# A float32 attention and two-MLP kernel: weight sums and splits moved from GpSimd to VectorE and ScalarE, y loads moved ahead of weight loads

## Chip, core and metric

One core of a Trainium2 chip. The metric is device time in microseconds, the median of several executions of one program. All values are float32; every product is made from split operands.

## What is computed

```python
# x: (8, 8, 512, 64), state: (8, 8, 32, 64)   (batch, head, token, width)
xread = softmax(x @ state.T / 8) @ state          # 8 batches x 512 tokens
sread = softmax(state @ x.T / 8) @ x              # 8 batches x 32 state tokens
x = concat([xread, sread], axis=2)                # as rows: 4608 tokens x 512
x = relu(x @ w_in) ** 2 @ w_out                   # 512 -> 2048 -> 512
out = ((x @ w1) * (x @ w2)) @ w3 @ w_out2         # 512 -> 1024 -> 1024 -> 512
```

## The kernel before

A float32 operand is split into two parts that TensorE takes at full rate: `hi`, a copy rounded to float32r (made by ScalarE), and `lo`, the whole minus `hi` (made by VectorE). A product is three matmuls, hi x hi, hi x lo, lo x hi.

The work has three stages.

Start: `w3 @ w_out2` is folded into one matrix W', and state and `w_in` into a table G, both written to DRAM.

First block, once for each batch tile t = 0 to 7 of 512 tokens (GpSimd's stores of y mark the ends of the tiles), and once more, as tile `SR` with 256 columns, for all the state tokens. A tile has 16 chunks f of the hidden width. For each chunk TensorE makes `h(f)` in a PSUM bank, ScalarE takes the relu (L1050), VectorE squares it (`h_chunk`, L1315 to L1320), ScalarE rounds the square to `v_hi`, VectorE subtracts to get `v_lo` (`minus`), and TensorE adds `y(f)` into four PSUM banks. TensorE runs `h` two chunks ahead of `y`: its order is h(f+2), a piece of the next batch's attention in some chunks, y(f). Beside each chunk, in a slot written out by hand (`in_slot`, `attention_slot`, `tile_slots`), ScalarE and VectorE carry on the softmax of the next batch and split the next pieces of x and G, which SP loads into a ring of 8 buffers `raw`; SP issues a load when the piece that held the buffer 8 pieces earlier is split. A batch tile splits 16 such pieces. Chunk and tile counts gate everything through semaphores.

Second block: `(x @ w1) * (x @ w2) @ W'` with a Strassen-like scheme of 7 products on 2 x 2 blocks. Its weights are sums of blocks of `w1` and `w2`; each of the sums is split too, and stands in `s_dram` (`s_scratch`), 8 kinds for each of 4 groups. In the kernel before GpSimd makes all of these: `S_weights(g)` (L609 to L645) loads four blocks of 128 x 512 into `top_f`, and for each kind copies with rounding into `top[:, 5]` (L627), subtracts into `top[:, 6]` (L620), and stores both as one DMA of 512 KB (L631), waiting for the last store before it overwrites the pair; 4 more operations are sums. `S_weights(0)` to `(3)` stand behind the stores of y of tiles 1 to 4, so they run beside tiles 2 to 5.

Between the blocks, in tile `SR`, SP loads the second block's weights (`load_S`) as the buffers they go to come free, then y of tile 0 into `raw` (`load_y`, L521), then the first four rows of W' (`load_wp`, L524). VectorE makes the column sums of y (`T_sums`, in slot 9), and 7 sets of y columns are rounded and split in slots 10 to 13 (`set_slots`), the 8 rows of W' in slots 14 and 15 (`wp_slots`). W' rows 4 to 7 are loaded into the ring buffers of rows 0 to 3. The second block's first chunk needs all sets, the weights of groups 0 and 1, the relu of the last chunk of `SR`, and, from its fifth product on, ScalarE's copy `P1`, which stands behind the rounding of W' rows 4 to 7 in ScalarE's program.

Of the kernel before, what the change touches and what calls it, by code (L numbers as in the profile page):

```python
# [34 lines left out]
def build_program(nc, x_tok, x_T, state_T, moe_w_in, moe_w_out, moe2_w1, moe2_w2, w3_T, moe2_w_out, out):  # L35
# [21 lines left out]
    RAW_AT = 4736  # L57
    TOP_AT = 214144
# [8 lines left out]
    SHIFT = 80  # L67
# [15 lines left out]
    with ctx:  # L83
# [49 lines left out]
        top_f = nc.alloc_sbuf_tensor_at("top_f", [P, N_SETS, C], F32, offset=TOP_AT)  # L133
# [19 lines left out]
        def sr(a):  # L153
# [10 lines left out]
                      .rearrange("p (j k n) -> p j k n", j=N_SETS, k=2)[:, :, :, 0:HT] for t in (X_hi, X_lo))  # L164
# [14 lines left out]
        def rest_bank(m):  # L179
# [11 lines left out]
                v_rows + [raw_r[:, k] for k in range(3)]]  # L191

        def A_block(g, row, col):

            half, kk = g // 2, g % 2
            c = 2 * col + kk
            return (moe2_w1, moe2_w2)[row][c * P:(c + 1) * P, half * C:(half + 1) * C]
# [53 lines left out]
        S_step = sem("S_step")  # L251
        S_stored = sem("S_stored")
# [113 lines left out]
        set_slots = {10: [0], 11: [1, 2], 12: [3, 4], 13: [5, 6]}  # L366
# [104 lines left out]
        def _(sp):  # L471
# [10 lines left out]
            def tile(b, slot_lists, r0, i=0):  # L482
# [26 lines left out]
            with sp.Fori(0, (NB - 2) // 2) as i:  # L509
                tile(2 * i + 1, tile_slots, R_1, i)  # L510
                tile(2 * i + 2, tile_slots, R_1 + PT, i)
# [21 lines left out]
            sp.wait_ge(S_stored, 16 * 4 * KINDS)  # L533
# [46 lines left out]
        def _(pool):  # L580
# [6 lines left out]
            last.then_inc(bd_zero, 1)  # L587
            nc.gpsimd.memset(ident[:], 1.0).then_inc(ones_ready, 1)
# [20 lines left out]
            def S_weights(g):  # L609
                A11, A12, A21, A22, S3 = (top_f[:, k] for k in range(5))  # L610
                n = g * (4 + 2 * KINDS)
                stores = g * KINDS
                for dst, row, col in ((A11, 0, 0), (A12, 0, 1), (A21, 1, 0), (A22, 1, 1)):
                    pool.dma_start(dst, A_block(g, row, col)).then_inc(A_loaded, 16)
                pool.wait_ge(A_loaded, 16 * 4 * (g + 1))

                def total(dst, a, b, op):
                    nonlocal n
                    wait_for(pool, S_step, n)
                    nc.gpsimd.tensor_tensor(dst, a, b, op).then_inc(S_step, 1)  # L620
                    n += 1

                def split(src, j):
                    nonlocal n, stores
                    wait_for(pool, S_stored, 16 * stores)
                    wait_for(pool, S_step, n)
                    nc.gpsimd.tensor_copy(top[:, 5], src).then_inc(S_step, 1)  # L627
                    n += 1
                    total(top[:, 6], src, top[:, 5].bitcast(F32), ALU.subtract)
                    pool.wait_ge(S_step, n)  # L630
                    pool.dma_start(s_dram[g, j].rearrange("k p n -> p k n"), top[:, 5:7].bitcast(F32)).then_inc(S_stored, 16)  # L631
                    stores += 1

                split(A11, 0)
                split(A21, 7)
                total(S3, A11, A21, ALU.subtract)
                split(S3, 2)
                total(A21, A21, A22, ALU.add)
                split(A21, 3)
                split(A22, 5)  # L640
                total(A11, A21, A11, ALU.subtract)
                split(A11, 1)
                split(A12, 4)
                total(A12, A12, A11, ALU.subtract)
                split(A12, 6)  # L645

            store_y(0, S)
            for g in range(4):
                store_y(g + 1, S)
                S_weights(g)  # L650
            for t in range(5, NB):
                store_y(t, S)
# [306 lines left out]
        def _(act):  # L959
# [87 lines left out]
            def h_chunk(t, n, f):  # L1047
                act.wait_ge(h_full, KF * t + f + 1)
                wait_for(act, sq_done, KF * t + f - 1)
                nc.scalar.activation(t1[:, f % 2, 0:n], ps_h[:, f % 2, 0:n], ACT.Relu).then_inc(relu_done, 1)  # L1050
                wait_for(act, y_full, KF * t + f - 3)
# [3 lines left out]
            def first_block(t, n, in_slot, next_chunk, next_slot):  # L1055

                for f in range(2, KF):
                    h_chunk(t, n, f)
# [116 lines left out]
            with act.Fori(0, (NB - 4) // 2) as i:  # L1175
                b = 2 * i + 1
                slot_b1 = batch_slot(b + 1, 0, tile_slots, R_1 + PT, i)
                first_block(b, S, batch_slot(b, 1, tile_slots, R_1, i), h_of(b + 1, S), slot_b1)
                first_block(b + 1, S, slot_b1, h_of(b + 2, S),
                            batch_slot(b + 2, 1, tile_slots, R_1 + 2 * PT, i))  # L1180
# [16 lines left out]
        def _(dve):  # L1197
# [117 lines left out]
            def h_chunk(t, n, f):  # L1315
                dve.wait_ge(relu_done, KF * t + f + 1)
                relu = t1[:, f % 2, 0:n]
                tt(t2[:, f % 2, 0:n], relu, relu, ALU.mult).then_inc(sq_done, 1)
# [194 lines left out]
```

## Time and profile before

| | us |
|---|---|
| median of 3 runs | 1301.54 (1298.03 to 1304.68) |
| the profiled execution | 1298.76 |
| its span in the profile | 1297.2 |

```profile
span 1297.2 us, 19431 instructions
## 1 busy us (share of the span) xinstructions
PE 1248.2 (96%) x7177; PEld 1083.0 (83%) x7177; DVE 835.7 (64%) x1397; ACT 476.6 (37%) x904; POOL 147.3 (11%) x164
## 2 busy tenths in 40 slices
PE   8979999999999989899999989999999999999998
PEld 6657888877877768778888989999999999999998
DVE  6666877678686786876554465666566665757541
ACT  6565554534445344454444231212122121212111
POOL 1000000044262442610000000000000000000000
PEclk9988999999999999999999999999999999999999
```

Each digit is a slice of 32 us. PE is TensorE, DVE VectorE, ACT ScalarE, POOL GpSimd. GpSimd has work in slices 9 to 18. The second block fills slices 24 to 40.

### The profile page before, as it was taken

Reading aid. Unit: us, or ns where it says so; the run is one execution under the profiler, and the core shown is the slowest. Engines: PE = TensorE matmul, PEld = TensorE weight load, DVE = VectorE, ACT = ScalarE, POOL = GpSimd, SP = SyncE. Lnnn points to the kernel's source line nnn. Section 1 sums busy time; section 2 is a strip of 40 time slices with the busy share of each in tenths; the row PEclk is TensorE's granted clock in tenths of the full one; section 3 lists DMA queues with packets and bytes.
Section 4 is the critical chain, followed back from the end, with each engine's and each line's share of the span. In section 5 each row is a group of like instructions: output and inputs, shape, how many; then the busy total and the mean of one; then the engine's idle time right before and its main releaser. Section 6 shows DMA issues by size and latency. Waiting matters only on the chain.

```text
span 1297.2 us, 19431 instructions
## 1 busy us (share of the span) xinstructions
PE 1248.2 (96%) x7177; PEld 1083.0 (83%) x7177; DVE 835.7 (64%) x1397; ACT 476.6 (37%) x904; POOL 147.3 (11%) x164
## 2 busy tenths in 40 slices
PE   8979999999999989899999989999999999999998
PEld 6657888877877768778888989999999999999998
DVE  6666877678686786876554465666566665757541
ACT  6565554534445344454444231212122121212111
POOL 1000000044262442610000000000000000000000
PEclk9988999999999999999999999999999999999999
DMA  8986431143433434331123770101010101010210
GB/s 297 363 295 210 137 129 55 64 155 135 141 129 122 145 120 130 130 126 59 42 98 122 252 266 11 66 1 65 0 65 0 65 0 65 3 61 0 82 50 33
DMA packets 63092, 139.10 MB, mean 107 GB/s; under 512 B 5184, under 2 KB 6208, under 8 KB 63040
## 3 DMA queue, kind: packets, MB, share of 16 engines
q1 hardware_dynamic: 51680, 96.49, 22.2%
q0 software_dynamic: 11360, 41.95, 9.2%
q8 instruction: 29, 0.48, 0.1%
q14 instruction: 23, 0.19, 0.0%
HBM read 84.93 MB, written 53.48 MB: 107 GB/s over the span
## 4 chain that ended last, share of the span: by engine, by line
PE 80%; DVE 11%; DMA 3%; ACT 3%; issue 2%; SPq 0%; DVEq 0%; ACTq 0%; POOL 0%; POOLq 0%
PE ps_y L674 39%; PE ps_h L674 21%; PE ps_t L674 18%; DVE t L1201 3%; ACT v_hi L964 2%; DVE GA L1201 1%; DVE s L1201 1%; DVE v_lo L1201 1%; DVE aT_lo L1201 1%; DMA g_scratch<-g_extra 1%; DMA wp_scratch<-stage 1%; DVE x_lo L1201 1%; DMA raw<-y_scratch 1%; DMA g_scratch<-stage 1%; PE ps_h L733 1%
## 5 line engine op out<-in xcount | busy, mean ns | idle before, releaser
L964 ACT CAST v_hi<-t 128x512 fp32r<-128x512 f32 (+1 forms) x216 | 128.9, 597 | 538.4 <-DVE t L1201 533.8
L674 PE MATMUL ps_y<-v_hi,X_hi 128*128 128x512 f32 (+1 forms) x576 | 223.3, 388 | 25.4 <-DVE v_lo L1201 23.1
L1201 DVE TENSOR_TENSOR v_lo<-t,v_hi 128x512 fp32r<-128x512 f32 (+1 forms) x216 | 150.3, 696 | 147.9 <-ACT v_hi L964 147.9
L674 PE MATMUL ps_y<-v_lo,X_hi 128*128 128x512 f32 (+1 forms) x576 | 219.9, 382 | 0.0
L674 PE MATMUL ps_y<-v_hi,X_lo 128*128 128x512 f32 (+1 forms) x576 | 219.2, 381 | 0.0
L1201 DVE TENSOR_TENSOR t<-t 128x256 f32<-128x256 f32 (+1 forms) x272 | 160.9, 611 | 83.9 <-ACT t L1050 81.5
L674 PEld LDWEIGHTS ps_y<-v_hi,X_hi 128*128 128x128 f32 x576 | 109.7, 190 | 52.9 <-DVE v_lo L1201 31.1
L674 PEld LDWEIGHTS ps_y<-v_hi,X_lo 128*128 128x128 f32 x576 | 109.9, 191 | 21.0
L1050 ACT ACTIVATE t<-ps_h 128x512 f32<-128x512 f32 (+1 forms) x144 | 82.3, 572 | 119.9 <-PE ps_h L674 119.4
L674 PEld LDWEIGHTS ps_y<-v_lo,X_hi 128*128 128x128 f32 x576 | 109.9, 191 | 19.1
L1201 DVE TENSOR_TENSOR t<-t,ps_t 128x256 f32<-128x256 f32 (+1 forms) x132 | 72.6, 550 | 48.1 <-PE ps_t L674 34.3
L674 PE MATMUL ps_h<-aT_hi,GA 128*128 128x512 f32 (+1 forms) x288 | 95.7, 378 | 0.5 <-ACT g_extra L964 0.5
L674 PE MATMUL ps_h<-aT_hi,GB 128*128 128x512 f32 (+1 forms) x288 | 95.6, 377 | 0.0
L674 PE MATMUL ps_y<-v_hi,GB 128*128 128x512 f32 (+1 forms) x288 | 91.6, 382 | 0.4 <-DVE v_lo L1201 0.4
L674 PE MATMUL ps_y<-v_hi,GA 128*128 128x512 f32 (+1 forms) x288 | 91.5, 381 | 0.0
L1201 DVE TENSOR_TENSOR t<-t,ps_h 128x256 f32<-128x256 f32 x132 | 55.0, 417 | 56.2 <-PE ps_h L674 44.2
L1201 DVE TENSOR_TENSOR t<-ps_t,t 128x512 f32<-128x512 f32 x64 | 44.2, 691 | 44.5 <-PE ps_t L674 43.7
L964 ACT COPY t<-ps_h 128x256 f32<-128x256 f32 (+1 forms) x74 | 31.5, 426 | 85.7 <-PE ps_h L674 81.9
L674 PEld LDWEIGHTS ps_h<-aT_hi,GA 128*128 128x128 f32 x288 | 53.3, 188 | 11.2 <-ACT g_extra L964 0.9
L674 PEld LDWEIGHTS ps_h<-aT_hi,GB 128*128 128x128 f32 x288 | 53.5, 189 | 10.1
L674 PEld LDWEIGHTS ps_y<-v_hi,GB 128*128 128x128 f32 x288 | 53.3, 188 | 10.3 <-DVE v_lo L1201 0.6
L1201 DVE TENSOR_TENSOR X_lo<-raw,X_hi 128x512 fp32r<-128x512 f32 x66 | 45.3, 687 | 25.0 <-ACT X_hi L964 24.9
(232 smaller groups left out, 2885.2 us busy)
## 6 DMA issues: line engine op xcount, KB each, us to landing
raw<-g_scratch SPq DMA_DIRECT2D x64, 256.0 KB
s_scratch<-top POOLq DMA_DIRECT2D x32, 512.0 KB, 3.8
raw<-in_moe_w_in SPq DMA_DIRECT2D x32, 256.0 KB
raw<-in_x_T SPq DMA_DIRECT2D x32, 256.0 KB
raw<-in_x_tok SPq DMA_DIRECT2D x32, 256.0 KB
y_scratch<-stage POOLq DMA_DIRECT2D x8, 1024.0 KB, 5.5
raw<-y_scratch SPq DMA_DIRECT2D x8, 1024.0 KB, 5.3
out<-stage POOLq DMA_DIRECT2D x8, 1024.0 KB, 4.6
```

The lines of the kernel that those rows point to most:

```text
L674: mm = nc.tensor.matmul(dst, w, m, start=first and n == 0, stop=last and n == 2)
L733: last = nc.tensor.matmul(pair_banks(p)[:, par, :], w[half, 0, par, rows], m[half], start=n == 0, stop=n == 2)
L964: return nc.scalar.copy(dst, src)
L1050: nc.scalar.activation(t1[:, f % 2, 0:n], ps_h[:, f % 2, 0:n], ACT.Relu).then_inc(relu_done, 1)
L1201: return nc.vector.tensor_tensor(dst, a, b, op)
```

## The change

1. GpSimd's `S_weights` goes. In `h_chunk` of tiles 1 to 4 a call `S_part(f, i, kk)` stands between the square and the low part on VectorE, and between the relu and the rounding of the square on ScalarE. In chunks 2, 3, 5, 7, 8, 10, 11 and 13 ScalarE rounds one kind and VectorE subtracts; in chunks 4, 6, 9 and 12 VectorE makes one sum. Each group takes one tile.
2. Two pairs of buffers are used in turn (`parts`: `top[:, 5:7]` and two rows of `E_lo`). GpSimd stores each part on its own, so 64 DMAs of 256 KB in place of 32 of 512 KB, and ScalarE waits for the stores two kinds back before it overwrites, and for all of them in chunk 15.
3. The loads of the blocks of `w1` and `w2` go from GpSimd's queue to SP's, behind the fourth piece of a tile, and behind a wait for the last split of the group before.
4. In SP's program the load of y tile 0 and of W' rows 0 to 3 goes ahead of the wait for the stored weights and of all `load_S`. `T_sums` goes from slot 9 to slot 8 of tile `SR`, set 0 to slot 9, and set 3 to slot 11.

```diff
+        parts = [(top[:, 5], top[:, 6]), (E_lo[:, 6], E_lo[:, 7])]
+        A11, A12, A21, A22, S3 = (top_f[:, k] for k in range(5))
+        work = {2: (A11, 0), 3: (A21, 7), 5: (S3, 2), 7: (A21, 3), 8: (A22, 5), 10: (A11, 1), 11: (A12, 4),
+                13: (A12, 6)}
+        total = {4: (S3, A11, A21, ALU.subtract), 6: (A21, A21, A22, ALU.add), 9: (A11, A21, A11, ALU.subtract),
+                 12: (A12, A12, A11, ALU.subtract)}
...
-        set_slots = {10: [0], 11: [1, 2], 12: [3, 4], 13: [5, 6]}
+        set_slots = {9: [0], 10: [1], 11: [2, 3], 12: [4], 13: [5, 6]}
...
+                    if kk is not None and n == 3:
+                        sp.wait_ge(S_split, i * 2 * KINDS + kk * KINDS + 1)
+                        for dst, row, col in ((A11, 0, 0), (A12, 0, 1), (A21, 1, 0), (A22, 1, 1)):
+                            sp.dma_start(dst, A_block(i, kk, row, col)).then_inc(A_loaded, 16)
...
-            sp.wait_ge(S_stored, 16 * 4 * KINDS)
+            sp.wait_ge(piece_split, N_RING)
+            sp.wait_ge(y_stored, 16)
+            load_y(y_main[0])
+            sp.wait_ge(wp_stored, 16 * 2)
+            for k in range(4):
+                load_wp(k)
+            for stored_part in S_stored:
+                sp.wait_ge(stored_part, 16 * 4 * KINDS)
             load_S(0, 1, range(N_SETS))
...
-            sp.wait_ge(piece_split, N_RING)
-            sp.wait_ge(y_stored, 16)
-            load_y(y_main[0])
-            sp.wait_ge(wp_stored, 16 * 2)
-            for k in range(4):
-                load_wp(k)
...
+            def store_S(i, kk):
+                for n, j in enumerate(order_S):
+                    pool.wait_ge(S_split, i * 2 * KINDS + kk * KINDS + n + 2)
+                    dst = s_dram.rearrange("(h k) j s p n -> h k j s p n", k=2)[i][kk, j]
+                    for part in range(2):
+                        pool.dma_start(dst[part], parts[n % 2][part].bitcast(F32)).then_inc(S_stored[n % 2], 16)
...
+            def S_part(f, i, kk):
+                if f in work:
+                    n = order_S.index(work[f][1])
+                    if n == 0:
+                        act.wait_ge(A_loaded, i * 2 * 64 + (kk + 1) * 64)
+                    if n > 1:
+                        act.wait_ge(S_stored[n % 2], i * 32 * KINDS + (kk * KINDS // 2 + n // 2) * 32)
+                    if f > 4:
+                        act.wait_ge(S_total, i * 8 + kk * 4 + (f > 4) + (f > 6) + (f > 9) + (f > 12))
+                    copy(parts[n % 2][0], work[f][0]).then_inc(S_rounded, 1)
+                if f == 15:
+                    for stored_part in S_stored:
+                        act.wait_ge(stored_part, i * 32 * KINDS + (kk + 1) * 16 * KINDS)
...
+            def S_part(f, i, kk):
+                if f == 2:
+                    dve.wait_ge(A_loaded, i * 2 * 64 + (kk + 1) * 64)
+                if f in work:
+                    n = order_S.index(work[f][1])
+                    dve.wait_ge(S_rounded, i * 2 * KINDS + kk * KINDS + n + 1)
+                    tt(parts[n % 2][1], work[f][0], parts[n % 2][0].bitcast(F32), ALU.subtract).then_inc(S_split, 1)
+                if f in total:
+                    dst, a, b, op = total[f]
+                    tt(dst, a, b, op).then_inc(S_total, 1)
...
-                if f == 9:
+                if f == 8:
                     T_sums(0)
```

## Rows read from the trace of the kernel before

**Rows 1.** Who waited for whom: idle us in total, times, longest.

```profile
PE ps_y L674 <- DVE v_lo L1201: 23.5, 18, 2.9
```

**Rows 2.** Timeline, GpSimd, 150 to 700 us: start, us, engine, line, operation [idle before].

```profile
185.48 0.75 POOL L607 DMA_DIRECT2D y_scratch<-stage  x1 [73.84 <-DVE stage L1335]
257.49 0.75 POOL L607 DMA_DIRECT2D y_scratch<-stage  x1 [71.25 <-DVE stage L1335]
...
576.33 0.77 POOL L607 DMA_DIRECT2D y_scratch<-stage  x1 [19.63 <-DVE stage L1335]
```

**Rows 3.** Windows: busy us and instructions of each engine, clock, DMA share, GB/s.

```profile
180.00:252.00 72.00, 72.00 (x334) 60.07 (x333) 46.13 (x78) 35.62 (x68) 0.75 (x1) 1.00 0.23 74
...
330.00:410.00 80.00, 73.91 (x329) 60.07 (x328) 59.17 (x74) 33.84 (x67) 32.27 (x33) 0.98 0.39 131
```

**Rows 4.** Timeline, VectorE, 340 to 420 us.

```profile
355.68 2.46 DVE L1201 TENSOR_TENSOR t<-t 128x512 f32<-128x512 f32 x1
...
369.01 0.68 DVE L1201 TENSOR_TENSOR t<-t 128x512 f32<-128x512 f32 x1
```

**Rows 5.** Timeline, GpSimd, same stretch.

```profile
356.28 1.30 POOL L620 TENSOR_TENSOR top_f<-top_f 128x512 f32<-128x512 f32 x1
...
368.84 0.73 POOL L631 DMA_DIRECT2D s_scratch<-top  x1 [0.30 <-POOL top L620]
```

**Rows 6.** Timeline, VectorE, 183 to 262 us: chunks 6, 7 and 12 of tile 1.

```profile
205.74 0.68 DVE L1201 TENSOR_TENSOR t<-t 128x512 f32<-128x512 f32 x1
207.16 0.69 DVE L1201 TENSOR_TENSOR v_lo<-t,v_hi 128x512 fp32r<-128x512 f32 x1 [0.74 <-ACT v_hi L964]
...
211.41 0.69 DVE L1201 TENSOR_TENSOR v_lo<-t,v_hi 128x512 fp32r<-128x512 f32 x1 [1.02 <-ACT v_hi L964]
...
230.65 0.69 DVE L1201 TENSOR_TENSOR v_lo<-t,v_hi 128x512 fp32r<-128x512 f32 x1 [0.74 <-ACT v_hi L964]
```

**Rows 7.** Timeline, ScalarE, 183 to 262 us: relu and rounding of chunk 3.

```profile
189.15 0.60 ACT L1050 ACTIVATE t<-ps_h 128x512 f32<-128x512 f32 x1 [0.77 <-PE ps_h L674]
190.56 0.62 ACT L964 CAST v_hi<-t 128x512 fp32r<-128x512 f32 x1 [0.81 <-DVE t L1201]
```

**Rows 8.** Chain that ended last: start, us, what. Chunks 7 and 12.

```profile
216.23 2.72 PE ps_y L674 x12
...
237.60 2.72 PE ps_y L674 x12
```

**Rows 9.** Groups of instructions, GpSimd: count, busy us, mean ns, idle before, releaser.

```profile
L631 POOL DMA_DIRECT2D s_scratch<-top x32 | 23.5, 735 | 10.2 <-POOL top L620 10.2
```

**Rows 10.** Tile top: issue to landing of its stores.

```profile
DMA to landing us min/median/max: 3.1/3.8/7.4
```

**Rows 11.** Timeline, TensorE, 734 to 775 us: the three idle gaps.

```profile
743.67 0.39 PE L674 MATMUL ps_y<-v_hi,X_hi 128*128 128x256 f32 x1 [1.66 <-DVE v_lo L1201]
...
755.68 0.38 PE L674 MATMUL ps_h<-X_hi,E_hi 128*128 128x256 f32 x1 [1.68 <-ACT t L1050]
...
761.89 0.36 PE L674 MATMUL ps_h<-X_hi,E_lo 128*128 128x256 f32 x1 [3.12 <-ACT t L964]
```

**Rows 12.** Chain that ended last, 690 to 775 us: a y chunk and two transfers.

```profile
718.98 1.44 PE ps_y L674 x12
...
731.39 8.29 DMA raw<-y_scratch
...
754.54 4.27 DMA raw<-wp_scratch
```

**Rows 13.** Timeline, VectorE, 690 to 775 us.

```profile
715.52 0.69 DVE L1201 TENSOR_TENSOR GB<-raw,GB 128x512 fp32r<-128x512 f32 x1
...
731.90 0.43 DVE L1201 TENSOR_TENSOR v_lo<-t,v_hi 128x256 fp32r<-128x256 f32 x1 [0.53 <-ACT v_hi L964]
...
752.35 0.42 DVE L1201 TENSOR_TENSOR t<-t 128x256 f32<-128x256 f32 x1
```

**Rows 14.** Timeline, ScalarE, 690 to 775 us.

```profile
758.89 2.58 ACT L964 CAST GB<-raw 128x512 fp32r<-128x512 f32 x4 [1.74 <-DMA raw<-wp_scratch]
```

More of the change, by code:

```diff
@@ L57, in build_program @@
     RAW_AT = 4736
+    SHIFT = 80
     TOP_AT = 214144
@@ L132, in build_program @@
         top = sb("top", [P, N_SETS, C], F32R)
-        top_f = nc.alloc_sbuf_tensor_at("top_f", [P, N_SETS, C], F32, offset=TOP_AT)
+        top_f = nc.alloc_sbuf_tensor_at("top_f", [P, 5, C], F32, offset=TOP_AT)
         raw_r = nc.alloc_sbuf_tensor_at("raw_r", [P, 3, C], F32R, offset=RAW_AT + 4 * C * 4)
@@ L163, in build_program @@
         B_hi, B_lo = (t[:, 0:N_SETS + 1].rearrange("p k n -> p (k n)")[:, SHIFT:SHIFT + N_SETS * C]
-                      .rearrange("p (j k n) -> p j k n", j=N_SETS, k=2)[:, :, :, 0:HT] for t in (X_hi, X_lo))
+                      .rearrange("p (j k n) -> p j k n", j=N_SETS, k=2) for t in (X_hi, X_lo))
         y_in = raw[:, 0:KM, 0:TT].rearrange("p (h k) (s n) -> p h k s n", h=2, s=2)
@@ L191, in build_program, with A_block @@
                 v_rows + [raw_r[:, k] for k in range(3)]]
-        def A_block(g, row, col):
-            half, kk = g // 2, g % 2
+        parts = [(top[:, 5], top[:, 6]), (E_lo[:, 6], E_lo[:, 7])]
[4 more added lines that the diff above has]
+                 12: (A12, A12, A11, ALU.subtract)}
+        order_S = [j for _, j in work.values()]
+        def A_block(half, kk, row, col):
             c = 2 * col + kk
-            return (moe2_w1, moe2_w2)[row][c * P:(c + 1) * P, half * C:(half + 1) * C]
+            return (moe2_w1, moe2_w2)[row].rearrange("k (s n) -> s k n", n=C)[half][c * P:(c + 1) * P, :]
         st_zero = sem("st_zero")
@@ L508, in _ @@
             sp.wait_ge(g_stored_last, 16 * 2)
-            with sp.Fori(0, (NB - 2) // 2) as i:
-                tile(2 * i + 1, tile_slots, R_1, i)
-                tile(2 * i + 2, tile_slots, R_1 + PT, i)
+            with sp.Fori(0, (NB - 4) // 2) as i:
+                tile(2 * i + 1, tile_slots, R_1, i, 0)
+                tile(2 * i + 2, tile_slots, R_1 + PT, i, 1)
+            for b in range(NB - 3, NB - 1):
+                tile(b, tile_slots, R_1 + (b - 1) * PT)
             tile(7, tile7_slots, R_7)
@@ L607, in store_y @@
                 pool.dma_start(y_main[t] if n == S else y_rest, stage[:, :, 0:n]).then_inc(y_stored, 16)
[L609 to L645, printed above, removed]
@@ L652, in _ @@
+            store_y(0, S)
+            with pool.Fori(0, (NB - 4) // 2) as i:
+                for kk in range(2):
+                    store_S(i, kk)
+                    store_y(2 * i + kk + 1, S)
+            for t in range(NB - 3, NB):
                 store_y(t, S)
@@ L1050, in h_chunk @@
                 nc.scalar.activation(t1[:, f % 2, 0:n], ps_h[:, f % 2, 0:n], ACT.Relu).then_inc(relu_done, 1)
+                if group is not None:
+                    S_part(f, *group)
                 wait_for(act, y_full, KF * t + f - 3)
@@ L1053, in h_chunk, with first_block @@
                 copy(v_hi[:, f % 4, 0:n], t2[:, f % 2, 0:n]).then_inc(sq_hi, 1)
-            def first_block(t, n, in_slot, next_chunk, next_slot):
+            def first_block(t, n, in_slot, next_chunk, next_slot, group=None):
                 for f in range(2, KF):
-                    h_chunk(t, n, f)
+                    h_chunk(t, n, f, group)
                     in_slot(f)
@@ L1312, in _, with h_chunk @@
                         nc.vector.tensor_copy(stage[:, j, :], ps_y[:, j, :]).then_inc(wp_drained[1], 1)
-            def h_chunk(t, n, f):
+            def S_part(f, i, kk):
[8 more added lines that the diff above has]
+                    tt(dst, a, b, op).then_inc(S_total, 1)
+            def h_chunk(t, n, f, group=None):
                 dve.wait_ge(relu_done, KF * t + f + 1)
@@ L1318, in h_chunk, with first_block @@
                 tt(t2[:, f % 2, 0:n], relu, relu, ALU.mult).then_inc(sq_done, 1)
+                if group is not None:
+                    S_part(f, *group)
                 minus(v_lo[:, f % 4, 0:n], t2[:, f % 2, 0:n], v_hi[:, f % 4, 0:n], sq_hi,
                       KF * t + f + 1, sq_split)
-            def first_block(t, n, in_slot, next_chunk, next_slot):
+            def first_block(t, n, in_slot, next_chunk, next_slot, group=None):
                 for f in range(2, KF):
-                    h_chunk(t, n, f)
+                    h_chunk(t, n, f, group)
                     in_slot(f)
```

24 lines of the change are left out of this document (11 added, 13 removed).

## Prediction

> **What bounds the kernel now.** I read the waits first. TensorE is the engine that is nearly always busy, and in the whole span it waits 18 times, 23.5 us in all, for VectorE's low part `v_lo` before a y chunk [rows 1]. That is the largest wait of TensorE's own list, so the next question is where it falls.
>
> GpSimd's timeline gives the tiles their length, since it stores y at the end of each. From the end of tile 0 to that of tile 1 it is 257.49 - 185.48 = 72.0 us. From the end of tile 1 to that of tile 5 it is 576.33 - 257.49 = 318.84 us for four tiles, 79.7 each [rows 2]. The same instructions are issued on TensorE, VectorE and ScalarE in all five; what the four have more is `S_weights` on GpSimd. The excess is 318.84 - 4 x 72.01 = **30.8 us**.
>
> The windows say how it comes about. From 180 to 252 us TensorE is busy 72.00 of 72 us: the tile is bound by TensorE alone. From 330 to 410 us TensorE has 73.9 us of work in 80, and VectorE's busy time is 59.2 us against 46.1, though it ran 74 instructions and not more; GpSimd has 32.3 against 0.75 [rows 3]. So VectorE's instructions got longer. The timelines show one: a square of 128 x 512 that starts at 355.68 takes 2.46 us, and inside it GpSimd runs a sum of 1.30 us that starts at 356.28 [rows 4, 5]. The same square alone takes 0.68 us [rows 6]. VectorE loses GpSimd's whole instruction and a little more, and it does so in the chunks where it has no idle time to give.
>
> The Trainium skill has a rule for this (SBUF — State Buffer, "Who interferes with whom"): a VectorE instruction with two SBUF inputs and a GpSimd instruction that reads SBUF lock one another out, for the whole instruction. These rows agree: 2.46 against 0.68 + 1.30.
>
> The second place is tile `SR`. TensorE stands still three times there: 1.66 us before y(10), 1.68 us before the second block's first product, 3.12 us before its fifth [rows 11]. The chain of waits names two transfers: the load of y tile 0, issued at 731.39 and 8.29 us on its way, and the load of W' row 4, 4.27 us from 754.54 [rows 12].
>
> **Part 1: GpSimd's arithmetic goes.** 80 instructions of GpSimd that read SBUF (32 roundings, 32 subtractions and 16 sums) disappear, and with them the cause of the 30.8 us. The work comes back as 12 VectorE and 8 ScalarE instructions of 128 x 512 in each of tiles 1 to 4. What is their price?
>
> On VectorE a chunk has a hole between the square and the low part, because the low part waits for ScalarE's rounding: square 6 starts at 205.74 and takes 0.68, low part 6 starts at 207.16 [rows 6]. 205.74 + 0.68 + 0.69 = 207.11, so one more instruction of 0.69 us (the low part's duration, the same operation on the same shape) just fits, in chunk 6, which lies in the stretch where VectorE is otherwise full. ScalarE has the twin of this hole: the relu of chunk 3 ends at 189.15 + 0.60 = 189.75 and the rounding begins at 190.56, 0.81 us later, and one rounding takes 0.62 [rows 7]. The extra rounding ends at 190.37, before the square, which starts when the relu ends and takes 0.68, is over at 190.4. So the new subtraction finds its operand ready. I take a price of 0 on the chain relu, square, rounding, low part.
>
> The other bound is that the hole is of no use and each new instruction costs its full 0.69 us. Then VectorE falls behind in the full stretch, chunks 5 to 12. The tightest y is y(7): it starts at 216.23 [rows 8] and its low part ends at 211.41 + 0.69 = 212.10 [rows 6], a lead of 4.13 us; by then chunks 5, 6 and 7 have cost 2.07. At chunk 12 the eight instructions have cost 5.52, and the lead is 237.60 - (230.65 + 0.69) = 6.26 us [rows 6, 8]. Both leads hold, so TensorE does not wait at this bound either. It would from 6.26 / 8 = 0.78 us for each. VectorE's busy time becomes 46.1 + 12 x 0.69 = 54.4 of 72 us, ScalarE's 35.6 + 8 x 0.62 = 40.6 [rows 3, 6, 7]. So tiles 2 to 5 take 72.0 us, and tile 1, which gets the new work and has no GpSimd arithmetic even now, stays at 72.0. Part 1: **-30.8 us**, and from -30.8 up to about -29 if a chunk or two slip.
>
> **New waits of part 1.** (a) ScalarE waits for the stores two kinds back; its own rounding of the square, VectorE's low part and y are queued behind this. The nearest pairs are three chunks apart. A chunk is 12 y matmuls, 2.72 us [rows 8], and 6 h matmuls, half of that: 4.08 us, so 12.2 us. From the split to the landing of the second store: 0.3 us for GpSimd to wake [rows 5], one issue of 0.74 [rows 9] before the second, and 3.8 us to landing, at most 7.4 in 32 of them [rows 10], for twice the size. That is 4.8, at most 8.4; with some 2 us for relu, square and subtraction, 6.8 to 10.4 of 12.2. Hidden, with 1.8 us to spare at the worst. In chunk 15 the wait is two chunks behind, 8.2 us, and could hold ScalarE about 2 us at the worst; the lead of the last chunks, over 6 us as in chunk 12, covers that.
> (b) SP waits for the last split of a group, in chunk 13, before it issues four loads; queued behind it are the next tile's G pieces for slots 2 and 3 and all that follow. Released in chunk 13, it has five chunks, over 20 us, to chunk 2 of the next tile. Four issues at 0.74 at most and a landing, taken as high as the 8.29 us of [rows 12], are 11.3 us. Both the G pieces and the blocks are there in time. Cost 0; if the cover is gone, it is a wait of the next tile's slot 2 for the rest.
> (c) GpSimd now issues 16 stores in a tile, 16 x 0.74 = 11.8 us at most [rows 9]. Do these hold VectorE as the arithmetic did? An issue of the old stores at 368.84, 0.73 us long, lies over a square at 369.01, and this takes 0.68 us [rows 4, 5]. So no.
>
> **Part 2: y ahead of the weights.** The last ring piece is split at 715.52 + 0.69 = 716.2 [rows 13]; from then on y can be loaded. Before, SP gets to it at 731.39. With the 8.29 us of [rows 12] it now lands by 724.5, and the column sums in slot 8, behind the low part that ends at 731.90 + 0.43 = 732.3 [rows 13], find it there. The weight loads move back by some 3 us of issue; they have until the second block's first product, at 755.68 - 1.66 - 1.68 = 752.3 [rows 11], so I take 0 for that. Four sums of 0.69 us end at 735.1. From there I lay the chunks on. TensorE needs 1.44 us for y [rows 12] and as much for h, 2.88 a chunk. VectorE needs 0.42 for the square, 0.53 of waiting, 0.43 for the low part [rows 13] and 0.69 for each set: 2.07 with one set and 2.76 with two, so it keeps up and TensorE decides. h(12) ends where the first gap begins, at 743.67 - 1.66 = 742.0, so h(14) ends at 747.8, and with 0.4 for the relu square 14 starts at 748.2 in place of 752.35 [rows 13], 4.1 us earlier. y(10) does not wait (1.66 gone), and the relu of chunk 15 is done before y(13) is (1.68 gone). The third gap stays almost whole: ScalarE's copy `P1` is behind W' rows 4 to 7, whose load is issued only when row 0 is split; that is 4.1 us earlier too and again takes 4.27 us [rows 12, 14]. TensorE resumes at 761.89 - 4.1. Part 2: **-4.1 us**. Bounds: nothing, if the reload of W' queues behind the weights that were held back and takes the 8.3 us of [rows 12] and more; -6.3, if it lands at once and only ScalarE's queue is left.
>
> **The sum.** -30.8 - 4.1 = -34.9 us. Against the profiled execution: 1298.8 - 34.9 = 1263.9. The median of the three runs lies 2.8 us above that execution, so I forecast 1301.5 - 34.9 = **1266.6 us**, a ratio of 0.973.
>
> **Rivals.**
> *Cover used up.* The new instructions cost more than the hole and the lead, since each waits for ScalarE in a stretch where ScalarE has the softmax exponentials as well. At 1.3 us for each (twice the duration), the eight of chunks 5 to 12 cost 10.4, 4.1 us over the lead, 16.6 us in four tiles: **1283**. For it: the lock-step of two engines in every chunk. Against it: both holes in rows 6 and 7 are there in every ordinary chunk.
> *The stores block as the arithmetic did.* GpSimd's issues, 11.8 us in a tile, stretch VectorE as 32.3 us of activity stretched it by 13 [rows 3]. If they were as harmful as the arithmetic itself, some 11 of the 13 us would come back, 85% of 30.8: gain 4.6 + 4.1, **1293**. The square at 369.01 speaks against it.
> The Trainium skill warns of the other direction (same page, the "DVE blocks DMA" trap): VectorE in a two-port mode keeps GpSimd from writing a transfer's descriptors, while `tensor_tensor` is inferred not to. If that held here, stores would land late and the last rival below begins; the issues in [rows 9] average 735 ns beside a busy VectorE, which is no sign of it.
> *The arithmetic is not the cause.* VectorE would be slowed by the transfers of those tiles, which stay: only part 2 remains, **1297**. The 1.30 us inside the 2.46 speaks against it.
> *Slower: the stores pace the tile.* Place: ScalarE's wait for the stores two kinds back, three such steps in a tile. With a time R from split to landing each step takes R + 2 in place of 12.2 us. Three steps cost 3 x (R - 10.2) less the lead of 4.1. The gain is used up at 8.7 us a tile, R = 14.5; at R = 16 it is 4 x 13.3 = 53 us: **1320**. R was at most 8.4 above, so it would have to double, through twice as many transfers in one queue.
>
> **How the numbers follow.** Forecast 0.83, cover used up 0.07, stores block 0.03, not the cause 0.03, stores pace 0.04. The forecast's own range: part 2 from 0 to -6.3 gives 1264 to 1271, the offset to the median (0 to 2.8) and the spread of the runs (about 3.3 to each side) make it 1260 to 1274. To cover 8 in 10 with some of the first rival: 1258 to 1280. About 0.5%, 6.5 us, is what a measurement can tell from no change: faster by more 0.93, within it 0.03, slower 0.04.
>
> **What would show it.** Right: stores of y 72.0 us apart throughout; VectorE's squares at 0.69 us in all tiles, none over 1; the new subtraction between square and low part with the low part still 1.42 to 1.44 us behind the square; of the three gaps only the last. Wrong: waits of TensorE for `v_lo` in tiles 1 to 4 (first rival), squares of over 1 us beside store issues (second) or without any (third), or ScalarE idle for `s_scratch` stores (fourth). The second block is assumed unchanged; if TensorE's clock fell there, the sum would be off by that.

## The result and the profile after

The changed kernel takes **1264.7 us** (median; 1262.0 to 1265.1) against 1300.8 of the kernel before in the same comparison, a ratio of 0.9716 with a 95% interval of 0.9687 to 0.9745. The forecast was 1266.6, 0.973. A second, longer comparison of the same kernel gave 1265.3 and 0.9725 (0.9712 to 0.9738). The profiled span is 1263.0 us, 34.2 less than before.

The page of the changed kernel, its totals. GpSimd is down from 147 us to 57, TensorE idles 24 us in place of 49, and VectorE does more instructions in less busy time.

```profile
span 1263.0 us, 19633 instructions
## 1 busy us (share of the span) xinstructions
PE 1239.3 (98%) x7177; PEld 1081.5 (86%) x7177; DVE 809.8 (64%) x1445; ACT 496.4 (39%) x936; POOL 56.6 (4%) x101
```

The lengths of the tiles, as in [rows 2]: GpSimd's timeline, start, us, engine, line, operation, and the idle time before in brackets. From the end of tile 1 to that of tile 5 it is now 546.31 - 259.13 = 287.2 us, 71.8 a tile, in place of 318.84; tile 1 took 72.2, tile 6 71.9. Tiles 2 to 4, which have new work, took 71.87 us each, tile 5, which has none, 71.58. The excess of the four tiles is gone: 31.7 us.

```profile
186.96 0.75 POOL L623 DMA_DIRECT2D y_scratch<-stage  x1 [73.87 <-DVE stage L1350]
...
259.13 0.76 POOL L623 DMA_DIRECT2D y_scratch<-stage  x1 [20.86 <-DVE stage L1350]
...
546.31 0.76 POOL L623 DMA_DIRECT2D y_scratch<-stage  x1 [70.83 <-DVE stage L1350]
618.17 0.75 POOL L623 DMA_DIRECT2D y_scratch<-stage  x1 [71.10 <-DVE stage L1350]
```

The windows that answer [rows 3] (us, then the busy time of PE, PEld, DVE, ACT and POOL with their instructions, granted clock, DMA share, GB/s): 72 us of tiles 1 and 2, with the new work. VectorE has 53.4 us of work in place of the 59.2 (in 80 us) of the disturbed and the 46.1 of the undisturbed stretch, and TensorE is busy in every one of the 72 us.

```profile
252.00:324.00 72.00, 72.00 (x334) 60.09 (x333) 53.44 (x90) 39.76 (x76) 9.41 (x17) 1.00 0.43 146
```

VectorE's timeline in tile 1 of the changed kernel, chunks 6, 7 and 12, beside [rows 6]. The new sum of chunk 6 (`top_f`) starts 0.60 us behind the square, and the low part 1.42 us behind the square, exactly the distance of before.

```profile
207.21 0.68 DVE L1203 TENSOR_TENSOR t<-t 128x512 f32<-128x512 f32 x1
207.81 0.68 DVE L1203 TENSOR_TENSOR top_f<-top_f 128x512 f32<-128x512 f32 x1
208.63 0.69 DVE L1203 TENSOR_TENSOR v_lo<-t,v_hi 128x512 fp32r<-128x512 f32 x1
...
212.60 0.69 DVE L1203 TENSOR_TENSOR v_lo<-t,v_hi 128x512 fp32r<-128x512 f32 x1
...
232.06 0.69 DVE L1203 TENSOR_TENSOR v_lo<-t,v_hi 128x512 fp32r<-128x512 f32 x1
```

ScalarE's timeline of chunk 3, beside [rows 7]: relu, new rounding into `E_lo`, rounding of the square. The last still begins 1.42 us behind the relu's start, against 1.41.

```profile
190.62 0.60 ACT L1050 ACTIVATE t<-ps_h 128x512 f32<-128x512 f32 x1 [0.77 <-PE ps_h L660]
191.12 0.61 ACT L950 CAST E_lo<-top_f 128x512 fp32r<-128x512 f32 x1
192.04 0.62 ACT L950 CAST v_hi<-t 128x512 fp32r<-128x512 f32 x1 [0.31 <-DVE t L1203]
```

In tile `SR` two of the three TensorE gaps of [rows 11] are gone. SP's timeline has the y load first, VectorE's has its column sums in slot 8 without a wait, TensorE's has the one gap that is left, and the chain of waits (start, us, what) has the reload of W' ahead of the gap and the first matmuls behind it.

```profile
686.20 0.39 SPq L535 DMA_DIRECT2D raw<-y_scratch  x1
...
689.60 4.48 SPq L532 DMA_DIRECT2D top<-s_scratch  x7
```

```profile
702.21 0.68 DVE L1203 TENSOR_TENSOR stT<-raw 128x512 f32<-128x512 f32 x1
...
718.19 0.42 DVE L1203 TENSOR_TENSOR t<-t 128x256 f32<-128x256 f32 x1
```

```profile
727.93 0.55 PE L660 MATMUL ps_h<-X_hi,E_lo 128*128 128x256 f32 x1 [3.04 <-ACT t L950]
```

```profile
720.39 4.46 DMA raw<-wp_scratch
...
727.93 1.62 PE ps_h L660 x6
729.55 2.06 PE ps_t L660 x12
```

From GpSimd's store of tile 6 to the fifth product it was 761.89 - 648.42 = 113.5 us and is 727.93 - 618.17 = 109.8: **3.7 us** less. The balance of the spans: +1.5 in the start and tile 0 (its store of y at 186.96 in place of 185.48; in the kernels below this moment lies between 185.2 and 187 whatever their edit), -31.7 for tiles 2 to 5, -3.7 for the state-token tile, and -0.3 in all the rest, together -34.2.

### The profile page after: what moved, and what is told of

The parts are those of the page before. It is cut to its first block, busy times and chain, and to the rows that moved or that the text cites. A ratio compares the mean times of both kernels' runs of the same rounds, so it can differ in the third digit from the quotient of the medians.

```text
span 1263.0 us, 19633 instructions
## 1 busy us (share of the span) xinstructions
PE 1239.3 (98%) x7177; PEld 1081.5 (86%) x7177; DVE 809.8 (64%) x1445; ACT 496.4 (39%) x936; POOL 56.6 (4%) x101
## 4 chain that ended last, share of the span: by engine, by line
PE 95%; DMA 3%; DVE 1%; ACT 1%; issue 0%; SPq 0%; POOL 0%; DVEq 0%; ACTq 0%; POOLq 0%
PE ps_y L660 48%; PE ps_h L660 27%; PE ps_t L660 18%; DMA g_scratch<-g_extra 1%; DMA wp_scratch<-stage 1%; PE ps_h L719 1%; DMA g_scratch<-stage 1%; PE ps_t L719 1%; PE ps_t L684 0%; DMA raw<-in_moe_w_in 0%; DMA raw<-wp_scratch 0%; ACT GB L950 0%; DVE t L1203 0%; ACT v_hi L950 0%; DVE X_lo L1203 0%
## 5 line engine op out<-in xcount | busy, mean ns | idle before, releaser
L660 PE MATMUL ps_y<-v_hi,X_hi 128*128 128x512 f32 (+1 forms) x576 | 219.6, 381 | 3.2 <-DVE stage L1292 3.2
L1203 DVE TENSOR_TENSOR v_lo<-t,v_hi 128x512 fp32r<-128x512 f32 (+1 forms) x216 | 143.0, 662 | 118.5 <-ACT v_hi L950 111.7
L1203 DVE TENSOR_TENSOR t<-t 128x256 f32<-128x256 f32 (+1 forms) x272 | 143.4, 547 | 103.2 <-ACT t L1050 100.2
L1203 DVE TENSOR_TENSOR t<-t,ps_h 128x256 f32<-128x256 f32 x132 | 54.9, 416 | 56.2 <-PE ps_h L660 44.2
L1203 DVE TENSOR_TENSOR t<-ps_t,t 128x512 f32<-128x512 f32 x64 | 44.2, 690 | 44.6 <-PE ps_t L660 43.8
```

The lines of the kernel that those rows point to most:

```text
L660: mm = nc.tensor.matmul(dst, w, m, start=first and n == 0, stop=last and n == 2)
L1203: return nc.vector.tensor_tensor(dst, a, b, op)
```

## Experiments

The theory has three steps: GpSimd's reading arithmetic, not its transfers, lengthened VectorE's instructions; the new instructions cost nothing, and would even at full price, because VectorE has a lead over TensorE; the y load is worth its two gaps by itself. Labels are set with what was expected, as it was written down before each run. The diffs are shortened. Every `gp_` kernel, extra_2 and one_pair ran once, so what is read from them are the lengths of tiles and instructions in the one trace; the kernel before took 1296 to 1305 us in the same comparisons.

### The two parts alone

```diff
# weights_alone: on the changed kernel
-            sp.wait_ge(piece_split, N_RING) ... load_y(y_main[0]) ... load_wp(k)   # ahead of load_S
+            (the same lines behind the last load_S(1, 0, ...), as before)
-        set_slots = {9: [0], 10: [1], 11: [2, 3], 12: [4], 13: [5, 6]}
+        set_slots = {10: [0], 11: [1, 2], 12: [3, 4], 13: [5, 6]}
-                if f == 8:
+                if f == 9:
                     T_sums(0)
```

> The changed kernel with its second part undone: the y load, the column sums and the sets stand where they stood before; only the weight sums and splits are on VectorE and ScalarE. Theory (two separate gains): tiles 2 to 5 at 71.9 us each, the two gaps of 1.7 us in the state-token tile back, so 3.7 us slower than the changed kernel: about 1268.5. Rival (the second part only pays once the first is in, or the other way round): a distance to the changed kernel well away from 3.7 us, under 1 or over 6.

Measured: 1268.3 us, 0.9749 (0.9732 to 0.9767), tiles 2 to 5 at 71.8 us. The gaps of the state-token tile are back on TensorE's timeline, the first longer than before (2.73 against 1.66), with the y load 9.35 us on its way. It is 3.6 us slower than the changed kernel, as the theory said, though the trace puts it otherwise: from the store of tile 6 to the fifth product it takes 731.79 - 616.88 = 114.9 us, 5.1 more than the changed kernel and 1.4 more than the kernel before, because the y load is issued as late as before and takes 9.35 us in place of 8.29.

```profile
713.42 0.38 PE L660 MATMUL ps_y<-v_hi,X_hi 128*128 128x256 f32 x1 [2.73 <-DVE v_lo L1203]
...
725.43 0.39 PE L660 MATMUL ps_h<-X_hi,E_hi 128*128 128x256 f32 x1 [1.68 <-ACT t L1050]
...
731.79 0.36 PE L660 MATMUL ps_h<-X_hi,E_lo 128*128 128x256 f32 x1 [3.27 <-ACT t L950]
```

The second part alone is the reverse of this diff, applied to the kernel before.

> The kernel before with the second part alone: y and the first rows of W' loaded ahead of the weights, column sums in slot 8; GpSimd still makes the weight sums. Theory: 3.7 us faster than before, about 1297, with tiles 2 to 5 still at 79.7 us, and of the three TensorE gaps of the state-token tile only the last left. Rival (the parts depend on each other): no change, within 1 us.

Measured: 1295.9 us, 0.9956 (0.9940 to 0.9973), so 3.5 to 7.8 us faster; tiles 2 to 5 at 79.8 us, and one wait of TensorE left between the blocks (who waited for whom: total, times, longest):

```profile
PE ps_h L674 <- ACT t L964: 3.2, 1, 3.2
```

From the store of tile 6 to the fifth product it takes 758.15 - 648.44 = 109.7 us, as in the changed kernel. The ratios multiply to 0.9749 x 0.9956 = 0.9706, against the 0.9716 of both. The intervals leave some 2 us open either way, and by the traces the second part is worth 3.8 us alone and 5.1 beside the first: two separate gains, independent to about 1.4 us.

### Arithmetic or transfers

```diff
# gp_transfers_only: on the kernel before
                 def total(dst, a, b, op):
-                    nc.gpsimd.tensor_tensor(dst, a, b, op).then_inc(S_step, 1)
+                    pass
                 def split(src, j):
-                    nc.gpsimd.tensor_copy(top[:, 5], src) ...; total(top[:, 6], ...)
+                    pool.wait_ge(h_full, KF * (g + 2) + (4, 6, 7, 9, 10, 11, 13, 14)[kind])
                     pool.dma_start(s_dram[g, j]..., top[:, 5:7]...)
```

> The kernel before, but GpSimd makes no sum, rounding or subtraction: it loads the blocks and stores the 32 pairs of 512 KB beside the same chunks of tiles 2 to 5, so the second block's weights are left out (it multiplies by zeros). Theory (GpSimd's arithmetic holds VectorE): tiles 2 to 5 at 72 us, VectorE's squares 0.69 us throughout, about 1269. Rival (the transfers or the issuing of the stores hold VectorE): tiles 2 to 5 near 79.7 us, squares over 1 us beside the issues, about 1300.

Measured: 1267.0 us, squares 0.677 to 0.693 us in all tiles. One of the tiles with all its loads and stores, as a window:

```profile
329.20:400.90 71.70, 71.70 (x333) 59.85 (x332) 46.06 (x79) 35.41 (x67) 8.67 (x13) 1.00 0.43 146
```

VectorE is at 46.1 us, as in the undisturbed tile, with a DMA share of 0.43. Loads, stores and their issuing, by themselves, do nothing to it. The rivals "the stores block" and "the arithmetic is not the cause" are out.

```diff
# gp_arithmetic_only: on the kernel before
-                for dst, row, col in (...): pool.dma_start(dst, A_block(g, row, col)) ...
                 def split(src, j):
+                    pool.wait_ge(h_full, KF * (g + 2) + (4, 6, 7, 9, 10, 11, 13, 14)[kind])
-                    pool.dma_start(s_dram[g, j]...)          # the 32 stores behind store_y(5, S)
```

> The kernel before, but GpSimd moves no data in tiles 2 to 5: the same 80 operations run there on zeros, released by the chunk count so that they are spread as before, and the 32 stores go out in tile 6. The second block's weights are left out. Theory: tiles 2 to 5 lengthened about as before, 77 to 82 us each, with squares of over 2 us; tile 6, which has only the issues of 32 stores, at 72. Rival (the transfers do it): tiles 2 to 5 at 72 us and tile 6 longer.

Measured: 1273.1 us, tiles 2 to 5 at 73.1 and tile 6, with the issues of the 32 stores, at 71.9. The direction is the theory's, the size is a miss: 73.1, not 77 to 82. VectorE's instructions are lengthened, by 54.0 - 46.3 = 7.7 us in a tile (the 46.3 is tile 1 of this kernel, with the same 79 instructions; the 44.2 that the next expectation names is tile 6, which has six fewer), but the tile grows only by 1.1.

So the loss is not in proportion to the lengthening. Either the moments of GpSimd's operations matter, or the transfers beside them.

```diff
# gp_arithmetic_late: on gp_arithmetic_only; gp_both_late: the same wait added to the kernel before
-                    pool.wait_ge(h_full, KF * (g + 2) + (4, 6, 7, 9, 10, 11, 13, 14)[kind])
+                    pool.wait_ge(h_full, KF * (g + 2) + (6, 7, 9, 10, 12, 14, 15, 16)[kind])
```

> As gp_arithmetic_only, with the eight groups of GpSimd operations released later in each tile (chunk counts 6, 7, 9, 10, 12, 14, 15, 16 in place of 4, 6, 7, 9, 10, 11, 13, 14), which is about where they ran in the kernel before. In gp_arithmetic_only VectorE's busy time rose by 10 us a tile (54.0 against 44.2) and the tile only to 73.1 us; in the kernel before it rose by 15.6 and the tiles to 79.7. Theory A (placement: what counts is how much falls into the stretch where VectorE is full, chunks 5 to 12, beyond its lead of 4 to 6 us): 75 to 80 us a tile. Theory B (the transfers of the kernel before are needed for its loss): 72 to 73.5 us again. The second block's weights are left out, as there.

> The kernel before, complete with GpSimd's loads, arithmetic and stores, with the eight groups released at the same chunk counts as in gp_arithmetic_late (6, 7, 9, 10, 12, 14, 15, 16). Only the transfers tell it from gp_arithmetic_late, whose tiles took 74.2 us. Theory A (the transfers do nothing; what raised the loss from 2.2 us a tile there to 7.7 in the kernel before is when GpSimd's operations start against VectorE's): 74 to 75 us a tile, about 1278. Theory B (the transfers add to the loss): 77 us or more, 1290 or more.

Measured: 1277.9 and 1280.6 us. The first gave tiles of 74.3 us, between its two theories (75 to 80, and 72 to 73.5), so it decides for neither; the second, 75.1, is next to the 74 to 75 of "the transfers do nothing" and below the 77 of its rival. Tile 3 of each kernel as a window, the kernel before first, then gp_arithmetic_only, gp_arithmetic_late and gp_both_late:

```profile
335.10:415.90 80.80, 74.71 (x333) 60.73 (x332) 59.85 (x79) 34.64 (x67) 32.26 (x33) 0.98 0.39 130
```

```profile
331.60:404.70 73.10, 72.19 (x334) 59.91 (x333) 53.95 (x79) 34.77 (x69) 25.62 (x22) 1.00 0.22 72
```

```profile
331.60:405.90 74.30, 72.67 (x334) 59.85 (x333) 56.17 (x79) 34.73 (x68) 25.93 (x21) 1.00 0.22 71
```

```profile
333.60:409.50 75.90, 73.75 (x335) 59.86 (x334) 58.28 (x79) 34.56 (x68) 31.97 (x34) 1.00 0.41 138
```

Against 46.3 us, VectorE is lengthened by 7.7, 9.9 and 12.0 us, and the four tiles take 73.1, 74.3 and 75.1 us on average, 1.1, 2.3 and 3.1 over 72.0. In the kernel before it is 13.6 us more, and the four take 79.7. The transfers, with GpSimd's waits for them, are worth 0.8 us a tile (74.3 to 75.1). The other 4.6 us (75.1 to 79.7) go with the moments at which GpSimd's groups start: the two kernels differ in nothing but one wait of GpSimd's per group. One difference can be seen: in the kernel before two squares in a row take 2.46 and 2.43 us (the first is in [rows 4]), while in the released kernels none is over 1.78 but a single one of 2.14 in gp_both_late. A square has the rounding, the low part and y behind it. Why 1.6 us more of lengthening costs 4.6 us more of tile was not taken apart any further and stays open.

### What in the arithmetic holds VectorE

```diff
# gp_memset_late: on gp_arithmetic_late
-                    nc.gpsimd.tensor_copy(top[:, 5], src)
+                    nc.gpsimd.memset(top[:, 5], 0.0)
-                    nc.gpsimd.tensor_tensor(dst, a, b, op)
+                    nc.gpsimd.memset(top[:, 5:7], 0.0); nc.gpsimd.memset(top[:, 4], 0.0)
```

> As gp_arithmetic_late, but each GpSimd operation is replaced by one that only writes SBUF: a rounding by a memset of 128x512, a sum or subtraction by memsets of 128x1024 and 128x512. GpSimd's busy time is about the same, 20 to 25 us a tile; the weights are left out. Theory (VectorE is held by GpSimd's reads of SBUF, since it reads two operands from there): VectorE's busy time back to 44 to 45 us a tile, squares 0.69 us, tiles at 72 us, the same as with no GpSimd work. Rival (any GpSimd activity on SBUF holds VectorE): VectorE's busy time 52 to 60 us, squares over 1 us.

Measured: 1270.3 us, tiles 2 to 5 at 71.8. GpSimd writes to SBUF for 22.1 us of the tile, and VectorE is at 46.3 us:

```profile
330.80:402.70 71.90, 71.90 (x334) 60.03 (x333) 46.27 (x79) 35.60 (x69) 22.07 (x34) 1.00 0.23 73
```

The same kernel's timelines, first VectorE's, then GpSimd's. A square of 0.68 us runs beside a memset of 0.96 us.

```profile
358.47 0.68 DVE L1204 TENSOR_TENSOR t<-t 128x512 f32<-128x512 f32 x1
```

```profile
357.97 0.96 POOL L619 MEMSET top<- 128x1024 f32 x1
```

These writes of GpSimd's are harmless; what holds VectorE is GpSimd reading SBUF. The Trainium skill says this (SBUF — State Buffer, "Who interferes with whom"): a VectorE instruction with two SBUF inputs contends with a GpSimd instruction that reads SBUF, and not with one that only writes it. The run agrees, 46.3 us against 56.2.

### The price of the new instructions

```diff
# work_behind_low_part: on the changed kernel, h_chunk of ScalarE and of VectorE
-                if group is not None:
-                    S_part(f, *group)
                 (rounding of the square)   /   minus(v_lo ...)
+                if group is not None:
+                    S_part(f, *group)
```

> The changed kernel with the new instructions behind the low part in place of in the hole before it, on both engines: the rounding behind v_hi on ScalarE, the subtraction or sum behind v_lo on VectorE. Then each costs its full 0.6 to 0.7 us of VectorE's time, 8 of them in chunks 5 to 12, 4.8 to 5.5 us. Theory (the lead of 4 us at chunk 7 and 6 us at chunk 12 covers this, as the second bound of the prediction says): tiles at 72 us, the same time as the changed kernel, 1264 to 1266. Rival (the hole is what makes the change free): tiles 1 to 4 at 74 us or more, 1273 or more.

Measured: 1264.4 us, 0.9712 (0.9694 to 0.9729): no difference from the changed kernel; tiles at 71.8 to 72.2 us. The lead is being used, though. The low part of chunk 12 and y(12) in this kernel, from VectorE's timeline and from the chain of waits:

```profile
234.44 0.69 DVE L1203 TENSOR_TENSOR v_lo<-t,v_hi 128x512 fp32r<-128x512 f32 x1 [0.74 <-ACT v_hi L950]
```

```profile
237.72 2.72 PE ps_y L660 x12
```

The lead is 237.72 - (234.44 + 0.69) = 2.6 us. In the changed kernel y(12) starts at 239.07, by its chain of waits below, and the low part ends at 232.06 + 0.69: 6.3 us, as before. So 3.7 us of the 6.3 are used up here, and nothing of them shows.

```profile
239.07 2.72 PE ps_y L660 x12
```

```diff
# extra_2: on the changed kernel, behind minus(v_lo ...) in VectorE's h_chunk
+                if group is not None and 5 <= f <= 12:
+                    for e in range(2):
+                        nc.vector.tensor_reduce(line[:, c:c + 1], t2[:, f % 2, 0:n], AXX, ALU.max)
```

> The changed kernel with two more VectorE instructions, maxima of 128x512 of 0.64 us each, behind the low part in each of chunks 5 to 12 of tiles 1 to 4: 16 x 0.6 = 10 us of work more a tile, outside the hole. Theory (the lead of VectorE over TensorE is about 6.3 us at chunk 12, and what exceeds it stops TensorE): tiles 1 to 4 at 75 to 76 us, 1276 to 1280 in all, with waits for v_lo in late chunks. Rival 1 (VectorE's busy share decides, 64 of 72 us): 72 us a tile, about 1265. Rival 2 (no lead is left in the changed kernel): all 10 us show, 82 us a tile, about 1305.

Measured: 1273.7 us; tiles 2 to 4 at 74.0, 2.1 over the changed kernel's 71.9, and tile 1 at 76.7. The direction is the theory's, the size is a miss (75 to 76 a tile, 1276 to 1280 in all): 16 x 0.6 = 9.6 us of work, less the lead of 6.3, would be 3.3. Rival 1 falls, since the tile grows with VectorE busy for 62 of its 74 us; rival 2 falls too. How the 2.1 us come about is not cleanly shown: in tile 2 TensorE waits 0.8 us for `v_lo` and 0.7 for a part of the attention, and ScalarE waits 2.84 us for stores in chunk 15. In tile 1, which takes 2.7 us more, that wait is the longest:

```profile
252.06 0.62 ACT L950 CAST v_hi<-t 128x512 fp32r<-128x512 f32 x1 [4.48 <-DMA s_scratch<-E_lo]
```

That is the wait of chunk 15 for the last stores, 4.48 us: when VectorE is late in chunk 13, the two chunks from there to the wait are not enough. The prediction's fourth rival has this place, and here it shows.

### The stores

```diff
# one_pair: on the changed kernel
-        parts = [(top[:, 5], top[:, 6]), (E_lo[:, 6], E_lo[:, 7])]
+        parts = [(top[:, 5], top[:, 6])] * 2
-                    if n > 1:
-                        act.wait_ge(S_stored[n % 2], i * 32 * KINDS + (kk * KINDS // 2 + n // 2) * 32)
+                    if n > 0:
+                        act.wait_ge(S_stored[(n - 1) % 2], i * 32 * KINDS + (kk * KINDS // 2 + (n - 1) // 2 + 1) * 32)
```

> The changed kernel with one pair of buffers for the parts in place of two, so ScalarE waits for the store of the kind just before. The rounding of a kind in the chunk after another (chunks 3, 8 and 11) then waits for a store that was issued under 1 us before it; a store lands 2.7 to 4.7 us after its issue, so ScalarE, and with it v_hi and v_lo, is held some 4 us in each. Theory (the lead of 4 to 6 us absorbs one such hold, not two in a row): tiles 1 to 4 at 73 to 75 us, 1268 to 1277 in all, ScalarE idle for s_scratch stores. Rival 1 (stores are hidden even so): 72 us, 1265. Rival 2 (every hold shows in full): 84 us a tile, about 1312.

Measured: 1272.3 us; tiles 1 to 4 at 72.2, 74.0, 77.0 and 72.7. Who waited for whom, one_pair:

```profile
ACT top L950 <- DMA s_scratch<-top: 57.1, 16, 7.3
```

ScalarE is held 57 us before the new roundings, and the four tiles together take 8.2 us more than in the changed kernel (the whole kernel 7.0 more than changed_again): the lead absorbs most holds, not all. The changed kernel has no such wait in its list; its second pair of buffers is what keeps the stores off the path.

### The gap that is left

```diff
# p1_first: on the changed kernel
-        wp_slots = {14: [0, 1, 2, 3], 15: [4, 5, 6, 7]}
+        wp_slots = {14: [0, 1, 2, 3]}
-            first_block(SR, NT, sread_slot, lambda f: ab_chunk(0, 0) if f == 0 else None, lambda f: None)
+            first_block(SR, NT, sread_slot, lambda f: ab_chunk(0, 0) if f == 0 else None,
+                        lambda f: [wp_round(k) for k in range(4, KG)] if f == 0 else None)
```

and the same with `wp_lower` on VectorE.

> The changed kernel once more, unedited, on the chip of this group, as the yardstick for the next one: 1262 to 1266.

> The changed kernel with the rounding and splitting of W' rows 4 to 7 moved behind the second block's first chunk, on ScalarE and VectorE, so that the copy P1 does not stand behind their load. Theory (the third TensorE gap is only this queueing; the rows are needed 4 chunks later): the 3.2 us gap before the fifth product shrinks to under 1 us, 2.5 to 3.2 us faster than the changed kernel, about 1261.5. Rival (something else is late next, VectorE's chain for the first chunk or the weights of groups 2 and 3): the gap moves elsewhere and the time is within 1 us of the changed kernel.

Measured: 1265.3 (1264.5 to 1266.1) for the changed kernel and **1259.6 us** (1257.5 to 1260.0) for p1_first, 0.9675 (0.9661 to 0.9689) of the kernel before. It is faster than the changed kernel by 5.7 us and not by the 2.5 to 3.2 expected. From the store of tile 6 to the fifth product it takes 724.60 - 618.04 = 106.6 us, where changed_again takes 727.16 - 617.26 = 109.9: 3.3 us less, and the gap is gone. Windows from 728 to 734 us, first changed_again, then p1_first:

```profile
728.00:734.00 6.00, 6.00 (x34) 6.00 (x34) 3.18 (x7) 0.62 (x1) 0.00 (x0) 0.59 0.55 208
```

```profile
728.00:734.00 6.00, 6.00 (x53) 6.00 (x52) 5.25 (x12) 3.52 (x8) 0.58 (x1) 1.00 1.05 390
```

The surplus is the clock. Behind its idle 3.19 us changed_again's TensorE is granted 0.59 on average from 728 to 734 us (a mix of the full 2.4 GHz and the half, 1.2), where p1_first has 1.00. By the two chains of waits, first changed_again's, then p1_first's, the same 42 matmuls take 1.62 + 2.56 + 3.63 = 7.8 us in the one and 0.71 + 1.41 + 2.88 = 5.0 in the other.

```profile
727.16 1.62 PE ps_h L660 x6
728.78 2.56 PE ps_t L660 x12
731.34 3.63 PE ps_y L660 x24
```

```profile
724.76 0.71 PE ps_h L660 x6
725.47 1.41 PE ps_t L660 x12
726.88 2.88 PE ps_y L660 x24
```

The gap and the clock make 3.3 + 2.8 = 6.1 us. The two spans differ by 5.2, with p1_first 0.8 us later at the end of tile 0, so next to nothing is left over. In the other profiled execution of the changed kernel, shown further up, the same 42 matmuls take 6.6 us, a loss of 1.6.

The gap does not bring the clock down every time. Thirteen of the profiled kernels have one of 3.0 to 3.4 us at this place. In eleven the granted clock is 0.50 for part of the 6 us behind it, and the 42 matmuls take 6.6 to 8.0 us. In two, extra_2 (3.04 us) and work_behind_low_part (3.10 us), it stays at 1.00, as this window of the latter shows:

```profile
728.00:734.00 6.00, 6.00 (x54) 6.00 (x53) 4.08 (x10) 1.64 (x4) 0.75 (x1) 1.00 0.87 279
```

What decides between the two stays open. It makes single executions of these kernels differ by up to 3 us, whatever their edit.

## Why the prediction was right, point by point

**What bounded the kernel.** Right. Four tiles of 79.7 us became 71.8, and without GpSimd's reading arithmetic there is no loss (gp_transfers_only, gp_memset_late). By itself, released at other moments, it cost 1.1 or 2.3 us of the 7.7; the whole loss was seen in no kernel but those with the arithmetic, the transfers and the old moments together. What the prediction did not see is that the loss depends steeply on where the lengthening falls: 7.7 us of it cost a tile 1.1 us, 13.6 us cost 7.7. For a change that removes all of it this made no difference. One reading was too smooth: 2.46 us was taken to agree with 0.68 + 1.30, which is 1.98. No row explains the other 0.48 us, and the square is recorded as starting 0.6 us before the sum that is said to hold it [rows 4, 5].

**Part 1, forecast -30.8, measured -31.7.** The 0.9 us more is the yardstick: the prediction took tile 1's 72.01 us for an undisturbed tile, and tiles 2 to 5 came to 71.8. The price of zero in the hole is what the timelines show, with the low part still 1.42 us behind the square. The second bound, full price and still no wait, was tested and holds (work_behind_low_part), with 2.6 us of lead left. With 9.6 us of further work the time does rise (extra_2), by 2.1 us a tile where the prediction's way of counting gives 3.3.

**The new waits.** (a) The stores two kinds back cost nothing; an issue of 256 KB takes GpSimd 0.54 us in place of the 0.74 assumed, and a store landed at most 8.4 us after its issue, later than the 7.4 taken as the most; ScalarE still waits for none. The weak spot was the one named, chunk 15. (b) SP issues the blocks and then the G pieces in time; TensorE does not wait at all from tile 1 to tile 6. (c) The issues leave VectorE alone, as the square at 369.01 had said [rows 4].

**Part 2, forecast -4.1, measured -3.7.** Two of three gaps went, as laid out chunk by chunk. The mis-sized term is small and has two halves, measured from the store of tile 6: square 14 came 103.9 - 100.0 = 3.9 us earlier, not 4.1, and the reload of W' took 4.46 us, not 4.27 [rows 12, 13]. The weight loads that were moved back keep the DMA engines busy throughout (DMA share 1.01 from 702 to 720 us) but land before they are needed, so the term of 0 for them held.

**The rivals.** *Cover used up*: out, the cover holds even at full price. *The stores block* and *the arithmetic is not the cause*: out by gp_transfers_only. The price of the first was worked out wrongly all the same: at the rate of [rows 3], 13 us for 32.3 of activity, 11.8 us of issues bring back 4.7 us and not 11, which makes 1278 and not 1293. *The stores pace the tile*: not here, but real; with one pair of buffers it costs the four tiles 8.2 us.

**The time.** 1266.6 forecast, 1264.7 measured. Part of the closeness is luck. For the profiled execution the sum gave 1263.9 and it took 1264.6, but only because the start came 1.5 us later, which no term foresaw; without that the sum would have been 0.8 us high. The 2.8 us between the profiled execution and the median of the runs, which the forecast carried over, is 0.1 us in the changed kernel; this alone is 2.7 us, more than the 1.9 us that the forecast was high. And how far TensorE's clock falls behind the gap that was left was no term at all, though it moves an execution by up to 3 us; it happened to cost about the same in the two that were profiled, 1.8 us before and 1.6 after.

## What to carry to other kernels

When a GpSimd operation runs beside a full VectorE, compare the duration of one VectorE instruction with and without it before counting GpSimd's time as free. Look for holes between dependent instructions of two engines that work in turn: one instruction fits there at no price, and the lead of the pair over the bounding engine (its start minus the end of what it waits for, chunk by chunk) says how much more may be added. A gap of TensorE can be worth more than its length: look at the granted clock behind it, in more than one execution.

## What the hardware showed beyond what was expected

- GpSimd memsets, 22 us a tile, left VectorE's squares at 0.69 us; with GpSimd's roundings and sums beside them single squares took 1.8 to 2.5 us.
- The same GpSimd operations cost a tile 1.1 to 7.7 us, by the moment at which they start and by the transfers beside them. In gp_arithmetic_only, released at a fixed point of the chunk, GpSimd's own sums took 1.62 us in the median against the 1.30 of [rows 5]; that part of the wait had then passed to GpSimd is likely, and not shown.
- TensorE gaps of 3.0 to 3.4 us were followed by a stretch at half the clock in eleven executions of thirteen, worth 1.6 to 3.0 us, and by full clock in two.
